# First attention head started by halves of the sequence, and the second head's copies put ahead of later loads

## What is computed

```
q_bits = (q @ proj > 0); k_bits = (k @ proj > 0)          # [B, H, S, 6]
mask   = q_bucket[:, :, :, None] == k_bucket[:, :, None, :]
scores = where(mask, q @ k.T / 8, -1e9); attn = softmax(scores)
x      = (attn @ v) as [1536 tokens, 512]
h      = x @ w1_in;  x = where(h > 0, h, exp(min(h, 0)) - 1) @ w1_out     # 512 -> 2048 -> 512
h      = x @ w2_in;  out = (s * max(h, 0)**2 + b) @ w2_out
```

## Time and profile before

| what | value |
|---|---|
| median of 3 runs (lowest, highest) | 759.06 us (757.96, 760.53) |
| profiled execution, its span | 757.57 us, 755.8 us |
| TensorE busy | 747.0 us, 99% of the span |
| VectorE, ScalarE, GpSimd busy | 393.6, 315.4, 311.4 us |
| TensorE's granted clock, mean | 1.0 of full speed |
| chain that ended last | TensorE 93%, GpSimd 3%, the others 1% each |
| attention, then two layers | to about 240 us, then to the end |

### The profile page before, as it was taken

The page is one execution under the profiler, slowest core; times in us unless marked ns, Lnnn a source line. Parts: engine busy times, 40 slices in busy tenths (PEclk is TensorE's granted clock), DMA queues, the critical chain, the costliest instruction groups (busy, mean ns, idle before and its releaser), DMA issues.

```text
span 755.8 us, 11775 instructions
## 1 busy us (share of the span) xinstructions
PE 747.0 (99%) x3760; PEld 643.0 (85%) x3760; DVE 393.6 (52%) x753; ACT 315.4 (42%) x612; POOL 311.4 (41%) x250
## 2 busy tenths in 40 slices
PE   8999999999999999999999999999999999999997
PEld 6999999999997888888888888888888888888886
DVE  6888888888884655342325232343234332343233
ACT  7888888888872121322123222222121212121211
POOL 6799988988998893000000666620000000000000
PEclk9999999999999999999999999999999999999999
DMA  6766666766423432000000233200001000010001
GB/s 172 177 157 129 154 146 138 154 135 140 125 69 87 128 124 84 1 1 1 0 1 0 83 96 98 92 20 1 0 1 56 0 0 0 0 56 0 0 0 56
DMA packets 44194, 50.67 MB, mean 67 GB/s; under 512 B 8244, under 2 KB 32644, under 8 KB 44164
## 3 DMA queue, kind: packets, MB, share of 16 engines
q1 hardware_dynamic: 43940, 50.06, 25.9%
q10 hardware_dynamic: 224, 0.22, 0.1%
HBM read 29.45 MB, written 3.19 MB: 43 GB/s over the span
## 4 chain that ended last, share of the span: by engine, by line
PE 93%; POOL 3%; DVE 1%; ACT 1%; DMA 1%; issue 1%; SPq 0%; POOLq 0%; DVEq 0%; ACTq 0%
PE acc L655 34%; PE h_ps L637 34%; PE pt_ps L602 7%; PE pv_ps L617 4%; PE pv_ps L618 4%; PE s_ps L588 4%; PE s_ps L589 4%; DMA all_inv<-inv_dram 1%; POOL pt_lo L434 1%; PE prep_ps L573 1%; PE prep_ps L572 1%; PE prep_ps L571 1%; ACT probs L747 1%; PE pv_ps L578 0%; POOL pt_hi L432 0%
## 5 line engine op out<-in xcount | busy, mean ns | idle before, releaser
L818 ACT ACTIVATE r_sb<-h_ps 128x512 f32<-128x512 f32 x96 | 57.4, 598 | 368.6 <-PE h_ps L637 368.6
L637 PE MATMUL h_ps<-xt_hi,wb_hi 128*128 (+1 forms) x288 | 112.1, 389 | 1.1 <-POOL wb_lo L476 1.1
L637 PE MATMUL h_ps<-xt_hi,wb_lo 128*128 (+1 forms) x288 | 112.0, 389 | 0.0
L637 PE MATMUL h_ps<-xt_lo,wb_hi 128*128 (+1 forms) x288 | 112.0, 389 | 0.0
L947 DVE TENSOR_SCALAR g_sb<-e_sb,sb_scale 128x512 f32<-128x512 f32 x48 | 27.8, 580 | 158.3 <-ACT e_sb L821 158.3
L945 DVE SCALAR_TENSOR_TENSOR g_sb<-e_sb,h_ps 128x512 f32<-128x512 f32 x48 | 33.0, 688 | 134.8 <-ACT e_sb L821 134.3
L849 DVE TENSOR_SCALAR_CACHE_REDUCE probs<-s_ps 128x768 f32<-128x768 f32 x96 | 91.9, 958 | 10.1 <-PE s_ps L589 7.2
L747 ACT ACTIVATE probs<-probs,row_min 128x768 f32<-128x768 f32 x96 | 90.0, 938 | 1.9 <-DVE probs L849 1.1
L602 PE MATMUL pt_ps<-ident_sb,probs 128*128 128x128 f32 x576 | 79.8, 274 | 1.2 <-DVE pt_lo L856 1.1
L953 DVE TENSOR_TENSOR g_lo<-g_sb,g_hi 128x512 fp32r<-128x512 f32 x96 | 73.1, 761 | 3.3
L602 PEld LDWEIGHTS pt_ps<-ident_sb,probs 128*128 128x128 f32 x576 | 68.4, 141 | 7.1 <-issue 2.4
(11 more groups left out here) (89 smaller groups left out, 1526.1 us busy)
## 6 DMA issues: line engine op xcount, KB each, us to landing
w_raw<-w_in_dram SPq DMA_DIRECT2D x32, 256.0 KB, 2.8
w_raw<-w_out_dram SPq DMA_DIRECT2D x32, 256.0 KB, 2.9
raw<-qk_dram SPq DMA_DIRECT2D x15, 384.0 KB, 8.7
qqk<-kt SPq DMA_DIRECT2D x15, 384.0 KB, 4.1
raw_v<-v_dram SPq DMA_DIRECT2D x16, 192.0 KB, 4.7
all_inv<-inv_dram SPq DMA_DIRECT2D x16, 192.0 KB
x_parts<-x_second SPq DMA_DIRECT2D x16, 192.0 KB, 6.8
out_dram<-o_sb SPq DMA_DIRECT2D x12, 256.0 KB, 2.1
```

Of the source, the lines that this page charges most:

```text
L637: last = mm(bank[:], w[a][:, kt * P:(kt + 1) * P], x[b], start=n == 0, stop=n == 3 * KT - 1)
```

## The change

Head 0's rows are loaded by halves of the sequence, each with keys and queries (SyncE the first 384 columns, ScalarE's queue the second). Each half has its own semaphores for landing, projection, high part, second place of the keys (`k0_twice`), low part and bits, and the scores of unit 0 wait by halves (`first_keys`). The low part of the second half of the keys moves from VectorE to GpSimd. The kept high queries `q0_high` move to `kt1[2]`, so that the wait for GpSimd stands at round_qk(2) and not at round_qk(1). In ScalarE's order round_qk(1) goes ahead of the rounding of `planes`, round_qk(2) from the end of unit 0 to the end of unit 1, round_qk(3) from unit 6 to unit 8. VectorE does the first `keep_scores` before `planes_lo`. In SyncE's order load_qk(2) goes behind copy_q_hi(1) and copy_q_lo(1); load_qk(3) and load_v(1) go behind copy_k(1) and copy_bits(1).

```diff
+FIRST_LATER = 2
...
-        q0_high = kt1[1][low, :]
+        q0_high = kt1[2][low, :]
@@ SyncE: load_qk(2), pair, and ahead of the pairs @@
-                    sp.wait_ge(z0_done, 1)
+                    sp.wait_ge(z0_done, 2)
                     sp.wait_ge(k0_hi, 2)
-                    sp.wait_ge(k0_lo, 1)
+                    sp.wait_ge(k0_twice, 2)
+                    for n in range(2):
+                        sp.wait_ge(k0_lo[n], 1)
...
                 copy_k(2 * i + 1)
                 copy_bits(2 * i + 1)
+                if i == 0:
+                    load_qk(3)
+                    load_v(1)
...
-            sp.dma_start(raw[0][top, :], qk[0, top, :]).then_inc(k0_in, 16)
-            sp.wait_ge(k0_in, 16)
+            sp.dma_start(raw[0][:, halves[0]], qk[0, :, halves[0]]).then_inc(rows0_in[0], 16)
+            sp.wait_ge(rows0_in[0], 16)
             load_qk(1)
             load_v(0)
             sp.dma_start(ident_sb[:], ident_in_d).then_inc(ident_in, 16)
-            load_qk(2)
             copy_q_hi(1)
             copy_q_lo(1)
-            load_qk(3)
-            load_v(1)
+            load_qk(2)
@@ GpSimd @@
-            pool.wait_ge(q0_in, 16)
-            for n in range(2):
-                cols = slice(n * HALF, (n + 1) * HALF)
+            for n, cols in enumerate(halves):
+                pool.wait_ge(rows0_in[n], 16)
+                if n == 1:
+
+                    pool.wait_ge(k0_hi, 2)
+                    nc.gpsimd.tensor_tensor(kt2[0][top, cols], raw[0][top, cols], kt1[0][top, cols].bitcast(F32),
+                                            ALU.subtract).then_inc(k0_lo[1], 1)
+                    pool.wait_ge(k0_lo[1], 1)
@@ TensorE: first_signs, scores, first_keys @@
-                pe.wait_ge(k0_in, 16)
-                pe.wait_ge(q0_in, 16)
                 for n in range(2):
-                    last = mm(s_ps[1][0:HEAD_ROWS, n, 0:HALF], planes0[:].rearrange("p w r -> p (w r)")[:, 0:HEAD_ROWS],
-                              raw[0][:, n * HALF:(n + 1) * HALF], start=True, stop=True)
-                last.then_inc(z0_done, 1)
+                    pe.wait_ge(rows0_in[n], 16)
+                    mm(s_ps[1][0:HEAD_ROWS, n, 0:HALF], planes0[:].rearrange("p w r -> p (w r)")[:, 0:HEAD_ROWS],
+                       raw[0][:, halves[n]], start=True, stop=True).then_inc(z0_done, 1)
...
+                    if isinstance(u, int) and u == 0:
+                        first_keys(n)
...
+            def first_keys(n):
+
+                pe.wait_ge(k0_hi, n + 1)
+                pe.wait_ge(k0_twice, n + 1)
+                pe.wait_ge(k0_lo[n], 1)
+                pe.wait_ge(k0_bits, n + 1)
...
-            pe.wait_ge(k0_hi, 2)
-            pe.wait_ge(k0_lo, 1)
-            pe.wait_ge(k0_bits, 1)
@@ ScalarE: round_qk, unit, and ahead of the units @@
-                if isinstance(head, int) and head == 1:
+                if isinstance(head, int) and head == 2:
                     act.wait_ge(q0_lo, 2)
...
-                start = isinstance(i, int) and i == 0 and k == 0
-
-                if rounded and not start:
+                first = isinstance(i, int) and i == 0
+
+                if rounded and not first or first and k == TILES + FIRST_LATER:
                     round_qk(2 * i + later, later % 2, operands(place, later), i + later % 2 + 1)
...
-                if start:
+                if first and k == 1:
                     round_qk(2, 0, 2, 1)
...
-            act.dma_start(raw[0][low, :], qk[0, low, :]).then_inc(q0_in, 16)
+            act.dma_start(raw[0][:, halves[1]], qk[0, :, halves[1]]).then_inc(rows0_in[1], 16)
...
-            act.wait_ge(k0_in, 16)
-            for rows in (top, low):
-                copy(kt1[0][rows, :], raw[0][top, :]).then_inc(k0_hi, 1)
-            act.wait_ge(q0_in, 16)
-            for n in range(2):
-                cols = slice(n * HALF, (n + 1) * HALF)
-                for q in (qt1, qt2):
-                    copy(q[0][top, cols], raw[0][low, cols]).then_inc(q0_hi, 1)
+            act.wait_ge(rows0_in[0], 16)
+            copy(kt1[0][top, halves[0]], raw[0][top, halves[0]]).then_inc(k0_hi, 1)
+            copy(qt1[0][top, halves[0]], raw[0][low, halves[0]]).then_inc(q0_hi, 1)
+            act.wait_ge(rows0_in[1], 16)
+            copy(kt1[0][top, halves[1]], raw[0][top, halves[1]]).then_inc(k0_hi, 1)
+            copy(qt2[0][top, halves[0]], raw[0][low, halves[0]]).then_inc(q0_hi, 1)
+            for cols in halves:
+                copy(kt1[0][low, cols], raw[0][top, cols]).then_inc(k0_twice, 1)
+            for q in (qt1, qt2):
+                copy(q[0][top, halves[1]], raw[0][low, halves[1]]).then_inc(q0_hi, 1)
+            round_qk(1, 1, 1, 1)
             act.wait_ge(planes_built, 3)
             copy(planes_hi[:], planes[:].rearrange("p n r w m -> p (n r w m)")).then_inc(planes_rounded, 1)
-            round_qk(1, 1, 1, 1)
@@ VectorE @@
-            tt(kt2[0][top, :], raw[0][top, :], kt1[0][top, :].bitcast(F32), ALU.subtract).then_inc(k0_lo, 1)
-            dve.wait_ge(z0_done, 1)
+            tt(kt2[0][top, halves[0]], raw[0][top, halves[0]], kt1[0][top, halves[0]].bitcast(F32),
+               ALU.subtract).then_inc(k0_lo[0], 1)
             k_at, q_at = slice(BIT_ROWS, HEAD_ROWS), slice(0, BIT_PAIR)
...
+            for n, cols in enumerate(halves):
+                dve.wait_ge(z0_done, n + 1)
+                to_bits(kt2[0][bit_rows, cols], s_ps[1][k_at, n, 0:HALF], k_at, C_THR0, C_AMP0).then_inc(k0_bits, 1)
+                to_bits(qt2[0][bit_rows, cols], s_ps[1][q_at, n, 0:HALF], q_at, C_THR0, C_AMP0).then_inc(q0_bits, 1)
+            dve.wait_ge(eps_ready, 1)
+            keep_scores(0, 0)
             dve.wait_ge(planes_rounded, 1)
...
-            dve.wait_ge(eps_ready, 1)
-            for k in range(AHEAD):
-                keep_scores(k, k)
+            keep_scores(1, 1)
```

More of the change, by code:

```diff
@@ L185, in build @@
         planes_split = sem("planes_split")
-        k0_in = sem("k0_in")
-        q0_in = sem("q0_in")
+        rows0_in = [sem(f"rows0_in{n}") for n in range(2)]
         z0_done = sem("z0_done")
         k0_hi = sem("k0_hi")
-        k0_lo = sem("k0_lo")
+        k0_twice = sem("k0_twice")
+        k0_lo = [sem(f"k0_lo{n}") for n in range(2)]
         k0_bits = sem("k0_bits")
@@ L242, in build @@
         out_stored = [sem(f"out_stored{n}") for n in range(KT)]
+        halves = [slice(n * HALF, (n + 1) * HALF) for n in range(2)]
         v_d = v.rearrange("h p t d -> h p (t d)")
```

## The result

The changed kernel is slower: 762.79 us median (762.40 to 764.70, 8 runs) against 760.65 for the kernel before in the 8 runs that stand beside it (757.96 to 762.79). The ratio is 1.0036, 95% interval 1.002 to 1.0053, where I had forecast a hair less than 1. The profiled execution took 762.80 with a span of 761.0, 5.2 more than the 755.8 of before. The profile of before was the fastest execution of its kernel, so the two profiles show the mechanism larger than the medians do (2.1 us).

The account below looks back on a forecast made before the run. The prediction took the kernel to be bound by TensorE, with idle time to save only in the first 19 us. -0.6 at the start + 0.2 at unit 8 = -0.4 us, median 758.7 from 759.06, range 757.2 to 760.4.

Parts of the forecast that it names:

- The start: Up to unit 0's scores copy on VectorE: front shift 0.75, the copy beginning at 8.9 instead of 9.64.
- Half 0: First load: lands at 3.9, bounds 0 and +0.7; an earlier landing excluded, as no row has 192 KB sooner than 3.1.
- The 0.6 of gain: End of the start: unit 3's transposes begin at 17.55 instead of 18.20, gain 0.6 us.
- rival A: Before exponential 3: ScalarE waits for head 2's rows; at a landing of 16.1, +1.0 us, median 760.1; chance 0.22.
- Head 1's copies ahead of the loads: SyncE's queue: two transfers fewer ahead of head 1's copies; TensorE didn't wait for them before, so saves nothing.
- Head 3's rounding at ScalarE and TensorE: Unit 8: 0.73 plus exponential 9 start where 0.28 was free; cost 0.2 us, bounds 0 and 0.45.
- Rival D: Head 3's rounding: its move costs its full 0.45 or more by GpSimd's backlog; -0.6 + 0.6 = 0; chance 0.1.
- The step that failed: SyncE's queue: copy_q_hi(3) waits some 2.5 us longer; readers of transfers behind come 5 us or more later, cost nothing.
- the chance of 0.04 for slower: Whole kernel: chances faster 0.04, same 0.92, slower 0.04, with 0.3% or 2.3 us as the bound of same.
- the gain of 0.4: Whole kernel: -0.6 at the start + 0.2 at unit 8 = -0.4 us, expected median 758.7; chance 0.45.
- -1.5 to +1.0 us: Whole kernel: all cases lie within this of before; -1.5 is front shift plus the rounding, +1.0 late head 2 rows.
- rows 4: Start of the profile before: trace rows giving GpSimd's 64x384 subtraction 1.59 beside VectorE's 1.29 subtraction, 1.00 alone.

Follow-up runs that it names:

- the better order: Changed kernel with head 3 rounded in unit 6, odd heads' loads behind the next wanted head's copies, even heads' copy_q_lo ahead of load_v: 757.01 us, ratio 0.9953.
- copy_q_lo alone: Changed kernel with head 3 rounded in unit 6 and copy_q_lo of even heads ahead of load_v, odd loads unmoved: 757.50 us, ratio 0.9975.
- the rounding alone: Kernel before with head 3 rounded in unit 8 instead of unit 6, no other edit: ratio 1.0073.
- before once more: Kernel before, unchanged, profiled a second time: 758.16 us, one run.
- the order on before: Kernel before with odd heads' loads (from head 5) behind the next wanted head's copies, even heads' copy_q_lo ahead of load_v: 758.22 us, ratio 0.9988.

## Why the prediction was wrong

**The start came out as worked out, with errors that cancelled and some luck.** Scores of unit 0 begin at 7.62 (worked out 7.9), round_qk(1) ends at 8.45 (8.3), split_qk(1) at 10.43 (10.45), unit 3's transposes start at 17.68 (17.55), and no rounding lies between exponentials 1 and 2. Half 0 landed at 3.5, earlier than the 3.9 below which I had excluded a gain. Two subtractions on VectorE were mis-sized: the keys' low part took 1.36 instead of 0.65, and planes_lo 1.03 instead of 0.2 to 0.3, so that exponential 1 came at 11.46 and not 11.13. Against that VectorE's first copy of scores began at 8.63 and not 8.9. The 0.6 of gain were 0.5.

How much of the 0.5 is the edit's is not shown. The other profiles with the old start have unit 3's transposes at 17.84, 17.91 and 18.10. Seven others with the halves have them between 17.56 and 18.04, but two, of the better order and of copy_q_lo alone, at 19.18 and 19.09. In those two the four matmuls of head 0's projection took 2.79 and 2.75 us instead of 1.49, at a granted clock of 1.00 as here, and unit 0's scores began at 9.07 and 9.01 instead of 7.62. The start of one and the same code so varies by more than the 0.6 that I worked out.

**Head 2 (rival A).** Its load went at 11.21, took 3.4 to land (14.6), and ScalarE rounded without idling at 14.80. The rival didn't come true; the landing was within the room I gave it.

**Head 1's copies ahead of the loads** I priced at nothing, since TensorE didn't wait for them in the one profile that I had. Three of four further profiles with the old order show 0.6 to 1.0 us of wait there (0.7 in the rounding alone, 1.0 in before once more, 0.6 in the order on before), so the part is worth something in executions unlike the one I read; no run here undoes it alone.

**Head 3's rounding at ScalarE and TensorE** cost 0.17 at unit 9, worked out as 0.2, and GpSimd's split_qk(3) started at 28.80 without a wait. Rival D did not come true either.

**The step that failed** is the last one of the same paragraph: that copy_q_hi(3) "waits some 2.5 us longer at SyncE", with the x move, load_v(3) and load_w(1) behind it, and that "their readers come 5 us or more later, so nothing". The wait was 3.2, and the copy was issued 2.5 us later than before (28.59 for 26.07), so the size was right; what was wrong is the nothing behind it. I looked at the readers of the three neighbours and stopped there. The list goes on: put_inv, whose landing SyncE itself waits for, get_inv, load_qk(5), copy_k(3), copy_bits(3). The last two have a reader without slack. The trace of before had the numbers: copy_k(3) was issued at 37.93 and took 6.8 to land, 44.7; copy_bits(3) was issued at 38.74, behind it; head 3's first scores ran at 46.09. So there was at most 1.4 us to spare. In the changed kernel copy_k(3) was issued 1.3 later (39.22) and took 8.6 instead of 6.8 to land, 47.8: 3.1 later in all, with DMA queues fuller by what had not been sent from 26 to 30 us. The copy's rows, before and after (duration of the issue in ns, start; then the landing), and head 3's first scores before:

```profile
L288 SPq DMA_DIRECT2D kt<-kt x1: 472/472/472, 37.9 to 37.9; - x1
DMA to landing us min/median/max: 6.8/6.8/6.8
46.09 0.34 PE L588 MATMUL s_ps<-kt,qqk 128*128 128x384 f32 x1
```

```profile
L294 SPq DMA_DIRECT2D kt<-kt x1: 473/473/473, 39.2 to 39.2; - x1
DMA to landing us min/median/max: 8.6/8.6/8.6
```

The rows of before I hadn't read: I had taken TensorE busy for 81.00 of 81 us as a sign of slack. It says only that every transfer came in time, not by how much.

None of my rivals had this place, and so the chance of 0.04 for slower and the upper end of 760.4 were too small. Of the 4.1 us between the forecast median (758.7) and the measured one (762.79), 1.6 are not the change's: the median of before itself is 760.65 in 8 runs, where the three that I had gave 759.06. The other 2.5 are the loss of 2.1 and the gain of 0.4 that didn't come. The price was also bounded too low in kind: I took -1.5 to +1.0 us as the reach of all cases, but a wait of 2.4 us brings the slow clock with it.

## What to carry to other kernels

When an instruction on a queue waits longer, go down that queue until the order meets another wait, and check the reader of each transfer on the way, the last ones above all. A busy TensorE hides how narrowly its data arrive: take issue, landing and first use of each copy from the trace and write down the difference. Put transfers with a near reader ahead of those with a far one, both in the issuing engine's order and thereby in the DMA queues; here that was worth more than a faster start.

## What the runs showed of the hardware

The same subtraction of 128x96 on VectorE took 0.26 us in the kernel before, with GpSimd idle, and 1.03 in the changed one, beside GpSimd's 128x768 subtraction (8.60 to 10.43). Both read two SBUF operands:

```profile
9.03 0.26 DVE L915 TENSOR_TENSOR planes_lo<-planes,planes_hi 128x96 fp32r<-128x96 f32 x1
```

```profile
8.60 1.83 POOL L429 TENSOR_TENSOR qqk<-raw,kt 128x768 fp32r<-128x768 f32 x1 [0.43 <-ACT kt L757]
...
9.52 1.03 DVE L934 TENSOR_TENSOR planes_lo<-planes,planes_hi 128x96 fp32r<-128x96 f32 x1
```

GpSimd's instruction took its usual 1.83 here; it was VectorE that paid, and I had counted the sharing only for GpSimd. The other runs say when. In ten profiles this subtraction began while a subtraction of GpSimd was running, 0.2 to 1.0 us before that one's end; it took 0.32 to 1.09 and ended 0.11 to 0.12 after GpSimd's in every one. Where GpSimd was idle (both profiles of before, the order on before) it took 0.26. The rows so fit an instruction that waits until the one begun earlier has ended. In rows 4 the order is the other way round: VectorE's subtraction runs from 4.80 to 6.09, GpSimd's begins at 5.35 and takes 1.59 instead of 1.00, ending 0.85 after it. It was the later one that paid, in both directions. The GPSIMD Engine Reference of the Trainium skill (Key points) names the two-operand case as one of contention; that the cost can fall on VectorE is this trace's.

After 2.4 us without a matmul TensorE's granted clock reads 0.50 from 49 to 52 us, and in the kernel with the rounding alone, after 2.8 us, from 49 to 55. With the wait filled by matmuls it reads 1.00.

The first 192 KB landed by 3.50, in rows of 1536 bytes over all partitions, where rows of 3072 bytes over half of the partitions had landed at 3.9. This holds in every profile here: 3.30 to 3.52 in the ten with halves, 3.92 to 4.00 in the four without.
